# Masks by sign operations, activations and W2 parts at other places of the slot

## The reference

```
scores = scale * q @ k.T
kth    = 32nd largest of each row;  scores below kth -> -1e9
attn   = exp(scores - max) / (sum + 1e-9);  x = attn @ v
h = x @ w_in;  g = h (h >= 1), 0 (h <= -1), (h+1)^2/4 between;  x = g @ w_out
h = max(x @ w2_in, 0);  out = h*h @ w2_out
```

## Time and profile before

| | us |
|---|---|
| median of 3 runs | 1258.61 (1258.48 to 1259.35) |
| the profiled execution's own time | 1258.23 |
| its span | 1256.4 |
| TensorE busy | 1193.2 (95%) |
| VectorE busy | 851.6 (68%) |
| ACT busy | 799.7 (64%) |
| GpSimd busy | 749.2 (60%) |
| TensorE's weight loads busy | 1128.0 (90%) |
| mean granted TensorE clock | 0.975 |

### The profile page before, as it was taken

How to read it: one execution, slowest core, us unless ns; L and a number is a source line. 1 busy time by engine, 2 the same in 40 slices (tenths; PEclk the granted TensorE clock), 3 DMA queues, 4 the chain that set the end, 5 groups by cost and what they waited for, 6 DMA issues and landing times.

```text
span 1256.4 us, 24445 instructions
## 1 busy us (share of the span) xinstructions
PE 1193.2 (95%) x8760; PEld 1128.0 (90%) x8760; DVE 851.6 (68%) x1884; ACT 799.7 (64%) x1788; POOL 749.2 (60%) x620
## 2 busy tenths in 40 slices
PE   6878889999989999999999999999999999999998
PEld 3667889998889999999999999999999999999997
DVE  7999999999877799999999987868730111110000
ACT  7887666776756666767766665666554665554443
POOL 6767787878767767767666766656652222222222
PEclk9767999999989999999999999999999999999999
DMA  6766978568879932334458831456349300870000
GB/s 250 282 252 223 337 278 301 198 233 301 288 265 367 383 128 97 126 109 142 135 174 299 291 120 39 150 176 208 101 148 369 145 35 4 314 287 18 18 17 17
DMA packets 94920, 239.53 MB, mean 191 GB/s; under 512 B 7760, under 2 KB 46672, under 8 KB 82512
## 3 DMA queue, kind: packets, MB, share of 16 engines
q1 hardware_dynamic: 94800, 237.98, 53.1%
HBM read 166.12 MB, written 71.83 MB: 189 GB/s over the span
## 4 chain that ended last, share of the span: by engine, by line
PE 68%; POOL 12%; DVE 6%; ACT 6%; issue 5%; DMA 1%; SPq 1%; ACTq 0%; POOLq 0%
PE h_ps L613 20%; PE y_ps L634 14%; PE y_ps L628 12%; PE score_ps L613 6%; PE pv_ps L572 5%; POOL s_sb L1083 4%; PE tr_ps L545 4%; POOL prob L1088 4%; DVE top L920 3%; PE score_ps L510 3%; DVE rest L922 2%; POOL w_out L1074 1%; POOL kq_lo L1066 1%; POOL g_lo L1101 1%; PE pv_ps L584 1%
## 5 line engine op out<-in xcount | busy, mean ns | idle before, releaser
L1101 POOL TENSOR_TENSOR g_lo<-rg,g_hi 128x256 fp32r<-128x256 f32 x288 | 215.5, 748 | 407.4 <-ACT g_hi L823 227.9
L613 PE MATMUL h_ps<-xt_hi,w_in 128*128 128x256 f32 x1880 | 390.6, 291 | 2.0 <-DVE xt_lo L968 1.7
L613 PEld LDWEIGHTS h_ps<-xt_hi,w_in 128*128 128x128 f32 x1880 | 309.3, 191 | 4.3 <-issue 2.1
L920 DVE MAX8 top<-rest 128x8 f32<-128x576 f32 x432 | 304.5, 745 | 0.4
L613 PE MATMUL h_ps<-xt_lo,w_in 128*128 128x256 f32 x940 | 266.0, 283 | 0.0
L1083 POOL TENSOR_SCALAR s_sb<-s_sb,top 128x576 f32<-128x576 f32 x126 | 228.2, 1811 | 43.5 <-DVE top L920 43.5
L628 PE MATMUL y_ps<-g_hi,w_out 128*128 128x256 f32 x1152 | 231.8, 284 | 0.7 <-ACT ys L789 0.4
L922 DVE MATCH_REPLACE8 rest<-top,rest 128x576 f32<-128x576 f32 x288 | 211.5, 741 | 0.0
L634 PE MATMUL y_ps<-w_out,g_hi 128*128 128x512 f32 x576 | 203.8, 395 | 3.8 <-DVE w_out L1002 3.1
L1088 POOL TENSOR_TENSOR prob<-s_sb,prob 128x576 f32<-128x576 f32 x128 | 182.7, 1430 | 15.4 <-ACT s_sb L749 4.4
L628 PEld LDWEIGHTS y_ps<-g_hi,w_out 128*128 128x128 f32 x1152 | 189.6, 192 | 2.1 <-issue 0.6
(11 more groups left out here) (90 smaller groups left out, 2076.1 us busy)
## 6 DMA issues: line engine op xcount, KB each, us to landing
w_in<-w_scratch SPq DMA_DIRECT2D x32, 1024.0 KB, 6.5
w_out<-w_scratch SPq DMA_DIRECT2D x32, 1024.0 KB, 7.9
ks<-kq_scratch SPq DMA_DIRECT2D x46, 576.0 KB, 6.0
qs<-kq_scratch SPq DMA_DIRECT2D x152, 128.0 KB, 4.2
w_scratch<-w_in SPq DMA_DIRECT2D x16, 1024.0 KB, 8.2
w_scratch<-w_out SPq DMA_DIRECT2D x16, 1024.0 KB, 8.1
v_sb<-in_vv_dram SPq DMA_DIRECT2D x48, 325.0 KB, 5.9
stage<-in_w_dram SPq DMA_DIRECT2D x24, 512.0 KB, 4.6
```

The source lines that it names most:

```text
L613: last = pe.matmul(h_bank(k), wi[:, f // 2, w, m, cols], x[:, m, :], start=(m == 0 and n == 0), stop=(m == KT - 1 and n == 2))
L920: dve.max(best, src[:, :]).then_inc(rank_step, 1)
L1101: pool.tensor_tensor(g_lo[k % 2][:, :], g_sb[k % 2][:, :], g_hi[k % 2][:, :].bitcast(F32), ALU.subtract).then_inc(g_lo_done, 1)
```

## The change

- Sign operations make the masks up to SIGNED = 18 in place of 9 (in the code's counting, the masks used in slots 10 to 18 too). The second pair stands behind the curve of position 3n.
- On ACT, `curve_at(3n)` now comes ahead of `hi_at(3n - 1)` in every slot, with a wait on g_hi_done in `curve` for layer 2.
- On VectorE, activations stand behind operation 0 (3n-1, of the slot before), behind operation 2 (3n) and behind operation 4 (3n+1). The totals come one operation later in slots 2 and 3.
- VectorE's W2 parts stand in the slot after, behind operation 2. W2_PER_SLOT makes the W2 blocks in slots 19 to 27, through four stages: the other two are kq_lo and kq_hi, so the tenth load of kq waits until all W2 parts are done.
- Three preparations go from slots 28, 30 and 32 to 29, 31 and 33.

```diff
-SIGNED = 9
+SIGNED = 18
-PREP_SLOT = (-1, 1, 3, 5, 7, 10, 12, 15, 17, 28, 30, 32, 38, 41, 44, 47)
+PREP_SLOT = (-1, 1, 3, 5, 7, 10, 12, 15, 17, 29, 31, 33, 38, 41, 44, 47)
+IDLE_KQ = sum(s < 18 for s in PREP_SLOT)
-W2_PER_SLOT = (1, 2, 2, 1, 2, 2, 1, 2, 2, 1)
+W2_PER_SLOT = (1, 2, 2, 2, 2, 2, 2, 2, 1)
 def stage_at(i):
-    return i % 4 if i < WBLOCKS else i % 2
+    return i % 4
 def stage_of(i):
-            return (stage[0], stage[1], xr, ys)[stage_at(i)]
+            if i < WBLOCKS or stage_at(i) < 2:
+                return (stage[0], stage[1], xr, ys)[stage_at(i)][:, :]
+            return (kq_lo, kq_hi)[stage_at(i) - 2][:, 0:2 * MODEL].bitcast(F32)
 def load_kq(at):                                        # SP
+                if at == IDLE_KQ:
+                    for i in range(2):
+                        sp.wait_ge(w_lo_done[i], WBLOCKS)
 def stage_block(i):                                     # SP
-                if i >= WBLOCKS:
-                    sp.wait_ge(w_lo_done[i % 2], i // 2)
-                elif i >= 4:
+                if i >= 4:
                     sp.wait_ge(w_lo_done[i % 2], i // 2 - 1)
+                if i >= WBLOCKS and stage_at(i) >= 2:
+                    sp.wait_ge(restacked, 16 * 3 * IDLE_KQ)
 def curve(k):                                           # ACT
                 if k >= 2 and JOBS[(k - 2) // FT][0] == 1:
                     act.wait_ge(g_done, CURVED[k - 2] + 1)
+                elif k >= 2:
+                    act.wait_ge(g_hi_done, k - 1)
 def slot(n):                                            # ACT
-                if 0 < n <= SIGNED:
-                    for t in range(2):
-                        keep_by_sign(n - 1, t)
+                signs = 0 < n <= SIGNED
+                if signs:
+                    keep_by_sign(n - 1, 0)
                 x_at(n)
+                curve_at(q)
+                if signs:
+                    keep_by_sign(n - 1, 1)
                 hi_at(q - 1)
-                curve_at(q)
 def slot(n):                                            # VectorE
                 both(0)
+                activate_at(3 * n - 1)
...
                 both(1)
...
-                at(3 * n)
-                behind = 1 if n < UP_POS[0] // 3 else 0
-                for op in (2, 3, 4):
+                read_at(3 * n)
+                behind = 2 if n < RAW_SLOTS else 1 if n < UP_POS[0] // 3 else 0
+                for op in (2, 3, 4, 5, 6):
                     if past and op == 2 + behind:
                         add_to_total(n - 2)
                     if past and op == 3 + behind:
                         invert_total(n - 2)
+                    if past and op == 4 + behind:
+                        scale_pv(n - 2)
                     if op == 4:
-                        if past and not behind:
-                            scale_pv(n - 2)
-                        at(3 * n + 1)
+                        read_at(3 * n + 1)
                     both(op)
-                if past and behind:
-                    scale_pv(n - 2)
-                both(5)
-                both(6)
-                at(3 * n + 2)
-                for i in range(2 * WBLOCKS):
-                    if W_SLOT[i] == n:
-                        split_w(i)
+                    if op == 2:
+                        activate_at(3 * n)
+                        for i in range(2 * WBLOCKS):
+                            if W_SLOT[i] == n - 1:
+                                split_w(i)
+                    if op == 4:
+                        activate_at(3 * n + 1)
+                read_at(3 * n + 2)
```

More of the change, by code:

```diff
@@ L132, in stage_at @@
 def stage_at(i):
-    return i % 4 if i < WBLOCKS else i % 2
-def staged_count(i):
-    return i // 4 + 1 if i < WBLOCKS else WBLOCKS // 4 + (i - WBLOCKS) // 2 + 1
+    return i % 4
 def own_bank(k):
@@ L380, in stage_block @@
             def stage_block(i):
-                if i >= WBLOCKS:
-                    sp.wait_ge(w_lo_done[i % 2], i // 2)
-                elif i >= 4:
+                if i >= 4:
                     sp.wait_ge(w_lo_done[i % 2], i // 2 - 1)
-                sp.dma_start(stage_of(i)[:, :], w_raw[i]).then_inc(w_staged[stage_at(i)], 16)
+                if i >= WBLOCKS and stage_at(i) >= 2:
+                    sp.wait_ge(restacked, 16 * 3 * IDLE_KQ)
+                sp.dma_start(stage_of(i), w_raw[i]).then_inc(w_staged[stage_at(i)], 16)
             def store_block(i):
@@ L689, in split_w @@
                 s, b = i // WBLOCKS, i % WBLOCKS
-                act.wait_ge(w_staged[stage_at(i)], 16 * staged_count(i))
+                act.wait_ge(w_staged[stage_at(i)], 16 * (i // 4 + 1))
                 if s:
@@ L693, in split_w @@
                     act.wait_ge(w_moved[b], 16)
-                act.activation(w_block(b)[:, 0, :], stage_of(i)[:, :], ACT.Copy).then_inc(w_hi_done, 1)
+                act.activation(w_block(b)[:, 0, :], stage_of(i), ACT.Copy).then_inc(w_hi_done, 1)
             def copy_scores(n, t):
@@ L978, in activate, with read_at, activate_at @@
                                              ALU.max).then_inc(g_done, 1)
-            def at(q):
+            def read_at(q):
                 if q in READ_AT:
                     split_x(READ_AT[q])
+            def activate_at(q):
                 if q in UP_AT:
@@ L1001, in split_w @@
                 b = w_block(i % WBLOCKS)
-                dve.tensor_tensor(b[:, 1, :], stage_of(i)[:, :], b[:, 0, :].bitcast(F32),
+                dve.tensor_tensor(b[:, 1, :], stage_of(i), b[:, 0, :].bitcast(F32),
                                   ALU.subtract).then_inc(w_lo_done[i % 2], 1)
@@ L1057, in _ @@
                 slot(n)
+            activate_at(ALONE - 1)
             for q in range(ALONE, END):
-                at(q)
+                read_at(q)
+                activate_at(q)
         @block.gpsimd
@@ L1073, in split_w @@
                 b = w_block(i % WBLOCKS)
-                pool.tensor_tensor(b[:, 1, :], stage_of(i)[:, :], b[:, 0, :].bitcast(F32),
+                pool.tensor_tensor(b[:, 1, :], stage_of(i), b[:, 0, :].bitcast(F32),
                                    ALU.subtract).then_inc(w_lo_done[i % 2], 1)
```

## The result

The changed kernel takes 1267.66 us (median of 4, 1267.63 to 1267.95); before, 1258.55. The ratio is 1.0074, interval 1.0062 to 1.0086: slower, by 9.1 us. Forecast were 1262.6 and a range of 1254 to 1269, so the sign and the range held and the forecast was 5 too low.

The account below looks back on a forecast made before the run. TensorE was taken as nearly full from 415.5 us on, earlier waiting for masks, GpSimd's products and the last W2 block. Terms 1.7 + 5.7 + 4.7 - 6.0 + 0.5 - 2.6 = +4.0 gave 1262.6 us, range 1254 to 1269.

Parts of the forecast that it names:

- Step 1: Slots 10 to 18, masks by sign operations on ACT: mask waits give way to ACT's work, +1.7 us in sum.
- the ring: Slots 11 to 16: ACT's cycle of work with the second sign pair sets the pace, 11.9 us per slot.
- Step 3: W2 parts, slots 19 to 27: GpSimd and VectorE parts in one slot delay the second product, +5.7 us.
- Step 4: hi_at(3n-1) behind curve_at(3n) on ACT: 0.25 us per layer-1 slot behind 34, nothing in layer 2, +4.7 us.
- rival (c): Layer-1 slots: activations meet g_lo, 21 x 0.3 us more, so 1268.9 us; chance 0.12.
- Step 5: Last W2 block, slot 28: 3.1 us wait and clock fall go, -6.0 us; preparation in 29 shows, +0.5.
- Step 6: Slot 50, activations later on VectorE: xt_lo wait shrinks from 1.68 to 0.4 us, clock fall goes, -2.6 us.

Follow-up runs that it names:

- ACT's order taken back: Changed kernel with hi_at(3n-1) ahead of curve_at(3n) on ACT again, VectorE's activations at their new places: 1258.47 us, ratio 0.9998 to the kernel before.
- the W2 plan alone: Kernel before with only the change's W2_PER_SLOT, PREP_SLOT and four stages, VectorE's W parts at the slot's end: 1256.73 us, ratio 0.9984.
- ACT's order alone: Kernel before with only curve_at(3n) ahead of hi_at(3n-1) on ACT, with its wait on g_hi_done: 1270.73 us, ratio 1.0098.
- the spread plan alone: Kernel before with only the W2 plan, its parts spread as (1, 2, 2, 1, 2, 2, 2, 2, 2): 1254.26 us, ratio 0.9963.
- candidate with the spread plan: Kernel before with W2 parts spread as (1, 2, 2, 1, 2, 2, 2, 2, 2) and VectorE's activations and totals at new places: 1249.49 us, ratio 0.9931.

## Why the prediction was right, and where it fell short

**Step 1** held: 11.87 against 11.9 a slot, +1.3 against +1.7. What it did not see is that the ring closes at 11.87 only with VectorE's new order.

**Step 3** was too dear by 2.4. Over a plain slot (12.67 in layer 1, 12.5 in layer 2), slots 21 to 23 cost 7.4 where I had 7.5, and slots 24 to 27 4.0 where I had 6.4. Against the kernel before, the rise is almost all slot 23, 3.5. Timeline of GpSimd and VectorE, slot 21:

```profile
247.99 0.91 POOL L1111 TENSOR_TENSOR g_lo<-rg,g_hi 128x256 fp32r<-128x256 f32 x1
248.88 2.69 POOL L1093 TENSOR_SCALAR s_sb<-s_sb,top 128x576 f32<-128x576 f32 x1
251.65 1.41 POOL L1098 TENSOR_TENSOR prob<-s_sb,prob 128x576 f32<-128x576 f32 x1
...
248.23 1.75 DVE L1009 TENSOR_TENSOR w_in<-stage,w_in 128x1024 fp32r<-128x1024 f32 x1
```

The product is done at 253.06, r + 7.4 (r is 245.65), not 8.0: the two activations of 0.4 that I put into GpSimd's chain lengthen its records by only 0.2 each (g_lo 0.91 for 0.74). The slot costs 1.97 above 12.67, not 2.5. On the overlap: from 247.99 to 251.57 the two engines did g_lo, compare and W part in 3.58 us, and singly these take 0.74, 1.73 and 1.21, 3.68. So here they ran one after the other in effect. In layer 2 they did not. Timeline of GpSimd and VectorE at the start of slot 26:

```profile
317.14 1.72 POOL L1093 TENSOR_SCALAR s_sb<-s_sb,top 128x576 f32<-128x576 f32 x1
318.94 1.58 POOL L1098 TENSOR_TENSOR prob<-s_sb,prob 128x576 f32<-128x576 f32 x1
...
318.02 1.21 DVE L1009 TENSOR_TENSOR w_in<-kq_hi,w_in 128x1024 fp32r<-128x1024 f32 x1
```

VectorE's part starts 0.9 us behind the compare, they overlap by 0.8 us, and both are as long as they are alone; slots 25 and 27 show the same. From 317.14 to 320.52 is 3.38 us, for work of 1.73, 1.43 and 1.21, 4.37. So nearly the whole part was hidden there, and I had hidden half of it. Four times the other half, 0.6, is an estimate of 2.4, which is what the step was too dear by. Nor does TensorE wait for the second product in slots 24, 25 and 27, as the step had it, but for the first, 0.6 to 0.7 us. The earlier trace rows decide nothing, for an operation that I had not looked at ran beside the same compare until 353.10, in VectorE's timeline of the kernel before:

```profile
350.60 2.50 DVE L968 TENSOR_TENSOR xt_lo<-xr,xt_hi 128x512 fp32r<-128x512 f32 x2 [3.90 <-ACT xt_hi L795]
```

The Trainium skill (SBUF — State Buffer, "SBUF: two separate sides") calls the shared port pair an exclusive lock that the first engine holds for its whole instruction while the other blocks. Slot 21's sum agrees with it, and slots 25 to 27 do not; there the measurement decides. Slot 23 cost 3.5 and not 2.5, since VectorE's xt_lo met the second product there, in its timeline and GpSimd's:

```profile
280.93 2.50 POOL L1098 TENSOR_TENSOR prob<-s_sb,prob 128x576 f32<-128x576 f32 x1
...
280.90 1.28 DVE L973 TENSOR_TENSOR xt_lo<-xr,xt_hi 128x512 fp32r<-128x512 f32 x2
```

**Step 4** is the step that failed, in its reach and not in its mechanism. In a plain slot it is right to the hundredth (12.91 or 12.92 against 12.67 + 0.25), and for slots 35 to 49 and 52 to 55 it gave +4.2 where +3.4 came. But slot 56, which it had at a quarter of a microsecond, cost 1.5; slot 34, which it left out, cost 1.1; and "Layer 2's curve is half a microsecond shorter, and there is nothing" was wrong in slots 71 to 73, 3.4 us together. Timeline of GpSimd and TensorE in slots 56 and 72:

```profile
714.26 0.73 POOL L1111 TENSOR_TENSOR g_lo<-rg,g_hi 128x256 fp32r<-128x256 f32 x1 [3.36 <-DVE top L925]
...
715.04 0.39 PE L629 MATMUL y_ps<-g_hi,w_out 128*128 128x256 f32 x1 [1.24 <-POOL g_lo L1111]
...
932.43 0.72 POOL L1111 TENSOR_TENSOR g_lo<-rg,g_hi 128x256 fp32r<-128x256 f32 x1 [3.61 <-ACT g_hi L826]
...
933.21 0.50 PE L635 MATMUL y_ps<-w_out,g_hi 128*128 128x512 f32 x1 [1.36 <-POOL g_lo L1111]
```

I had asked only when the turn of prob waits. Here down itself waits for g_lo(3n-1), and TensorE's `at` says why there:

```
first = k is not None and k % FT == 0
if first and q in DOWN_AT:
    down(DOWN_AT[q])
if k is not None:
    up(k)
```

At the first step of a job, down stands ahead of up, so the 1.5 us of an up-product no longer cover g_lo. That hurts where a job begins at position 3n+1: 103, 169 and 217, in slots 34, 56 and 72 (+1.1, +1.5, +2.2), and nowhere else behind slot 34. With ACT's order taken back, slots 56 and 72 are as before, and slot 34 keeps 0.7, as with the W2 plan alone. That down's place ahead of up makes the difference is read from the code and from these waits; no run exchanges the two. In slots 71 and 72 there are also no scores left for TensorE, and it waits for the second product 1.05 and 0.51. The time was near rival (c)'s 1268.9, but not by its mechanism: slots 36 to 38 show 12.9, and with 0.3 more from activations that meet g_lo they would show 13.2. That the time fell inside the range is in part luck: step 3 was 2.4 too dear, while slots 34, 56 and 71 to 73 together cost 5.8 more than they were given.

**Step 5** held: -6.5 against -6.0; the clock's part is in it, since no window from 348 to 364 us falls below 1.00. The preparations cost 1.7 rather than 0.5; 1.0 of it is ACT's order again (0.7 without it).

**Step 6** was too large. The wait for xt_lo is gone, as the timeline of TensorE shows (against the earlier trace rows):

```profile
642.66 0.63 PE L546 MATMUL tr_ps<-ident,prob 128*128 128x128 f32 x4 [1.05 <-POOL prob L1098]
...
646.72 0.36 PE L614 MATMUL h_ps<-xt_hi,w_in 128*128 128x256 f32 x1
```

A wait for the product stands in its place, 1.05, and two for ACT behind it; with ACT's order taken back, slots 50 to 55 gain 2.0. But ACT's order alone, with VectorE's old places, has no wait for xt_lo here either: it waits 1.06 for the product, and its slots 50 and 51 take 22.8 us as in the changed kernel. So beside ACT's new order VectorE's places gained nothing here, and the 2.0 are theirs only with the old one. The clock's share is not certain either: with the spread plan alone the wait of 1.68 stayed, the granted clock did not fall, and slots 50 to 55 took 1.1 less.

## What to carry to other kernels

When an operation is moved behind another on one engine, follow its product to every reader, in every phase: the slots where the reader has least work ahead of it (the first step of a job, the tail) pay more than the steady ones. An order that costs a quarter of a microsecond a slot can undo what all the other parts gain, and exchanging two lines of one engine's queue is the cheapest run to make. Parts that feed one ring must be priced together: in slots 11 to 18 the signs cost 3.5 alone and 1.3 with VectorE's new places.

## What the runs showed of the hardware

How an elementwise operation of GpSimd and one of VectorE share their time depends on which starts when. Where VectorE's W part started 0.65 us ahead of GpSimd's compare (248.23) or 0.2 us behind it (242.40), the compare took 2.69 and 2.95 us instead of 1.73, longer by most or all of the part's 1.21. Where the part started 0.3 us behind the compare (candidate with the spread plan, at 266.43) or 0.5 us (ACT's order back, at 346.76), the compare kept its 1.72, and the part took 1.50 and 1.33. Started 0.8 or 0.9 us behind it (slots 25 to 27), both kept their length and ran together for 0.8 to 0.9 us. I take a stretched record to hold waiting; what decides between these cases stays open.

Up to slot 10 executions of like instructions differ by up to 2.3 us in length (r of slot 10 is 0.6 to 2.9 us later than in the profiled execution before), with granted clocks from 0.58 to 0.97 in 60 to 116 us, which do not follow the length (0.97 where r is 1.2 later, 0.66 where it is 0.8 later); what sets this stays open.
